# Attention, mixture of experts and MLP on one core: experts' results added to the tokens' rows in place, and the attention of four batches written out as one pipeline

## The reference

```python
# attention: B=4 batches, H=8 heads, S=576, D=64, stride 32
scores = q @ k.transpose(0, 1, 3, 2) / sqrt(D)
mask_local   = (rel >= 0) & (rel < 32)                  # heads 0..3
mask_strided = (rel >= 0) & (pos_k % 32 == pos_q % 32)  # heads 4..7
attn = softmax(where(mask, scores, -1e9)); x = attn @ v  # -> 2304 tokens x 512
# experts: E=8, D=512, F=1024
do_compute = (x @ w_skip) > 0
e_idx = argmax(x @ w_gate); gate_w = softmax(x @ w_gate)[e_idx]
x[do_compute] += gate_w * (relu(x @ w1[e_idx]) @ w2[e_idx])
# MLP, 512 -> 2048 -> 512
h = x @ w_in; out = maximum(0.01 * h, h) @ w_out
```

## Time and profile before

| | |
|---|---|
| median of 3 runs | 775.59 us (773.31 to 780.62) |
| the profiled execution | 770.11 us |
| its span, first to last instruction | 768.4 us |
| granted TensorE clock over the span | 0.970 |
| busy: PE, DVE, ACT, POOL | 94%, 36%, 32%, 24% |

### The profile page before, as it was taken

The page is one execution under the profiler, slowest core; times in us unless marked ns, Lnnn a source line. Parts: engine busy times, 40 slices in busy tenths (PEclk is TensorE's granted clock), DMA queues, the critical chain, the costliest instruction groups (busy, mean ns, idle before and its releaser), DMA issues.

```text
span 768.4 us, 12937 instructions
## 1 busy us (share of the span) xinstructions
PE 722.8 (94%) x4664; PEld 672.0 (87%) x4664; DVE 275.3 (36%) x589; ACT 242.0 (32%) x522; POOL 185.3 (24%) x190
## 2 busy tenths in 40 slices
PE   4999979894989999998999999999999999999997
PEld 3898879883989999997989999989998999899986
DVE  5757747657100000003332243233223323332222
ACT  3467656451111111123222322222222232223222
POOL 3120100102588777543000400130031004001000
PEclk9999989895899999999999999999999999999999
DMA  8473745772699999983000200030021003001001
GB/s 188 120 182 94 183 128 167 248 256 70 217 279 334 335 335 358 337 243 85 17 1 1 96 29 1 28 96 1 0 77 46 0 12 111 0 0 42 1 1 41
DMA packets 72441, 91.47 MB, mean 119 GB/s; under 512 B 26872, under 2 KB 47896, under 8 KB 72401
## 3 DMA queue, kind: packets, MB, share of 16 engines
q1 hardware_dynamic: 62289, 62.70, 27.7%
q0 software_dynamic: 9056, 28.23, 11.8%
q10 hardware_dynamic: 1056, 0.02, 0.1%
HBM read 73.91 MB, written 17.01 MB: 118 GB/s over the span
## 4 chain that ended last, share of the span: by engine, by line
PE 80%; SPq 10%; DMA 4%; issue 2%; DVE 2%; POOL 1%; ACT 1%; ACTq 0%; POOLq 0%; DVEq 0%
PE psum L1654 26%; PE psum L1673 26%; PE psum L1556 9%; PE psum L1572 8%; SPq L429 6%; SPq L424 2%; PE psum L1396 2%; DMA x_rows<-xo 2%; PE psum L1421 1%; PE psum L1512 1%; PE psum L1495 1%; SPq L414 1%; PE psum L1636 1%; DMA xg<-x_rows,idx 1%; PE psum L1582 1%
## 5 line engine op out<-in xcount | busy, mean ns | idle before, releaser
L1654 PE MATMUL psum<-x2h,wih 128*128 128x384 f32 x384 | 130.6, 340 | 1.9 <-DVE x2l L1316 1.9
L1334 DVE SCALAR_TENSOR_TENSOR g_act<-g_raw 128x384 f32<-128x384 f32 x96 | 53.6, 558 | 219.1 <-ACT g_raw L995 218.7
L1654 PE MATMUL psum<-x2h,wil 128*128 128x384 f32 x384 | 129.4, 337 | 0.0
L1654 PE MATMUL psum<-x2l,wih 128*128 128x384 f32 x384 | 128.9, 336 | 0.0
L995 ACT ACTIVATE g_raw<-psum 128x384 f32<-128x384 f32 x96 | 47.1, 491 | 235.0 <-PE psum L1654 235.0
L1673 PE MATMUL psum<-woh,g_l 128*128 128x512 f32 x288 | 114.0, 396 | 0.0
L1673 PE MATMUL psum<-wol,g_h 128*128 128x512 f32 x288 | 113.8, 395 | 0.0
L1673 PE MATMUL psum<-woh,g_h 128*128 128x512 f32 x288 | 112.2, 389 | 0.7 <-DVE g_l L1338 0.7
L1556 PE MATMUL psum<-xt,wring 128*128 128x160 f32 x512 | 82.6, 309 | 0.6 <-issue 0.6
L792 POOL DMA_INDIRECT out_dram<-o_sb,idxo x15 | 15.9, 1060 | 277.3 <-ACT o_sb L990 274.3
L1572 PE MATMUL psum<-hp,wring 128*128 128x160 f32 x512 | 78.5, 302 | 0.0
(11 more groups left out here) (197 smaller groups left out, 892.1 us busy)
## 6 DMA issues: line engine op xcount, KB each, us to landing
wring<-in_moe_w_dram SPq DMA_DIRECT2D x64, 512.0 KB, 9.8
q_st<-in_q_dram SPq DMA_DIRECT2D x8, 576.0 KB
k_st<-in_k_dram SPq DMA_DIRECT2D x8, 576.0 KB
x_sb<-x_rows SPq DMA_DIRECT2D x4, 1024.0 KB, 6.2
stage<-in_moe_w_in_dram POOLq DMA_DIRECT2D x4, 1024.0 KB, 10.1
stage<-in_moe_w_out_dram POOLq DMA_DIRECT2D x4, 1024.0 KB, 11.1
y_rows<-zrow POOLq DMA_DIRECT2D x7, 480.0 KB, 6.9
vs<-in_v_dram SPq DMA_DIRECT2D x20, 128.0 KB, 6.9
```

The source lines that it names most:

```text
L1334: dve.scalar_tensor_tensor(out=g_act[:, f % 2, :], in0=g_raw[:, f % 2, :], scalar=LEAK, in1=g_raw[:, f % 2, :], op0=ALU.mult, op1=ALU.max) ...
L1654: last = pe.matmul(bank[f % 2][:, 0:MT * P], wt[:, c, f * P:(f + 1) * P], xp[:, T.par, c, :], start=(c == 0 and n == 0), stop=(c == KD - 1 ...
```

## The change

**Attention.** The four batches are written out on all engines, with constant addresses and counts, and one rule for every batch: own chunks 8 to 15 two at a time ahead of groups 1 to 4 (`CH_AT`), the next batch's 0 to 7 ahead of groups 7 to 10 (`CH_NEXT`). The copies of a chunk (`chunk_copies`, both sides read in the order of the target) are the same text in both kernels. In batch 0, Q and K of the first four heads come as two pairs of heads, chunks 1, 3, 5, 7 are copied by DVE, V's first three loads stand ahead of the second half of Q and K, and that half is copied by POOL. Later DVE copies 9 and 13. POOL does all four copies into `q_in`/`k_in` of the later batches. The zeroing of half of `kt` moves from DVE to POOL. ACT waits for POOL's `zrow`, stores it as a row of zeros, and runs one exponential ahead of its first chunk; the split of the gate's weights moves behind group 1.

**Experts.** There is no `y_rows` and no zero fill. DVE multiplies a tile's result by the gate, adds it to the gathered rows `xg` (now two buffers) into `yr` (`x2_rows`), and POOL scatters `yr` into `x_rows` (`put_x`). The gates of all tiles come from three more groups of columns of the one-hot product at f = 8 of the first tile (before: 56 columns at f = 5, now 56 and 132). The next `x_turn` stands at f = 6, and the gather for it waits for `x2_rows` of the tile before. The sorted list holds only the token number, and DVE finishes it ahead of the one-hot forms. The MLP gathers one row instead of two; for the first 384 tokens it does so in POOL's last iteration.

```diff
@@ attention
-        CH_AT = {2: [12], 3: [13], 4: [14], 5: [15], 7: [0, 1], 8: [2, 3], 9: [4, 5], 10: [6, 7]}
-        ON_DVE = {9, 11}
+        CH_AT = {1: [8, 9], 2: [10, 11], 3: [12, 13], 4: [14, 15]}
+        CH_NEXT = {7: [0, 1], 8: [2, 3], 9: [4, 5], 10: [6, 7]}
+        def on_dve(b, n):
+            return n % 2 == 1 if b == 0 and n < 8 else n in (9, 13)
...
-            with sp.Fori(0, B - 2) as b:
-                batch(b, True, True)
-            batch(B - 2, False, True)
-            batch(B - 1, False, False)
...
+            pool.memset(kt[:, :, 2:4, :], 0.0).then_inc(s_kz, 1)
             step(pool.memset(zrow[:, :], 0.0))
...
+            act.wait_ge(s_cst, POOL_ZROW)
+            act.dma_start(x_flat[NONE:NONE + 1, :], zrow[:, :]).then_inc(s_zd, 16)
...
-                    if s_ in (6, 8) and not last:
-                        act.wait_ge(s_tq, len(CH) * b + len(CH))
-                        act.wait_ge(s_qs[1], 16 * b + 32)
-                        to, what = heads_in(q_in, q_st, 1)
...
-            act.wait_ge(s_wg, 32)
-            act.activation(wgs[:, :, 0:E + 1], wg[:, :, :], ACT.Copy).then_inc(s_wgh, 1)
+            act.wait_ge(s_vz, 1)
+            act.activation(warm[0:STRIDE, :], vs[0:STRIDE, 0, 0, 0:1], ACT.Exp)
             act.wait_ge(s_vz, 3)
...
@@ PE, attention
-            head(0)
-            with pe.Fori(0, B - 1) as b:
-                rest(b, False)
-                head(b)
-            rest(B - 1, True)
+            for b in range(B):
+                for g in range(NG):
+                    for n in CH_AT.get(g, []):
+                        chunk(b, n)
+                    for n in CH_NEXT.get(g, []):
+                        if b + 1 < B:
+                            chunk(b + 1, n)
+                    if g in (0, NL):
+                        copied(b, 15 if g else 7)
+                    scores(b, g)
+                    if NG * b + g >= 2:
+                        probs(*divmod(NG * b + g - 2, NG))
+                    if NG * b + g >= 3:
+                        values(*divmod(NG * b + g - 3, NG))
@@ POOL, experts
             for i in range(2 * NU):
-                pool.wait_ge(s_xt, 2 * (i + 1))
-                gather_x(i + 1)
+                if i == 0:
+                    pool.wait_ge(s_xt, 2)
+                    gather_x(1, 1)
+                else:
+                    if i == 1:
+                        pool.wait_ge(s_zd, 16)
+                    pool.wait_ge(s_x2r, 2 * i)
+                    if i + 1 < E:
+                        gather_x(i + 1, (i + 1) % 2)
+                    put_x(i - 1)
...
                 if i == 0:
-                    pool.wait_ge(s_tok_o, 1)
+                    pool.wait_ge(s_tok_o, 2)
+                if i == 2 * NU - 1:
+                    pool.wait_ge(s_srt, 16)
+                    indices(0)
+                    gather_rows(s_gm)
                 stage_split(i)
-                if i < ZPARTS:
-                    pool.dma_start(fill_rows(ZEARLY + ZPART * i, ZPART),
...
+                if i:
+                    put_done(i - 1)
@@ DVE, experts
+            def x2_rows(i, par, at_=2):
+                dve.wait_ge(s_yt, i * 2 + 2)
...
+                dve.wait_ge(s_yf, i + 1)
+                for hf in range(2):
...
+                    dve.scalar_tensor_tensor(out=yr[:, hf, :], in0=bank[at_ + hf][0:HALF, :],
+                                             scalar=gate2[:, hf:hf + 1], in1=x_, op0=ALU.mult,
+                                             op1=ALU.add).then_inc(s_x2r, 1)
@@ PE, experts
-                    if f == 3:
+                    if ahead and f == (3 if first else 6):
...
-                    if first and f == 5:
+                    if first and f == 8:
...
+                            last = pe.matmul(GATE_O.rearrange("p k h -> p (k h)"), row_o[:, t, :],
+                                             gate_o[:, t, :, :].rearrange("p k h -> p (k h)"),
                                              start=(t == 0), stop=(t == NT - 1))
```

More of the change, by code:

```diff
@@ L464, in x_load @@
+            qk_load(sp, 0, 1, k, k_st, s_ks[1])
+            for g in range(3, NL):
+                v_load(sp, 0, g)
+            qk_next(1, 0)
+            for g in range(NL, NG):
+                v_load(sp, 0, g)
+            qk_next(1, 1)
             def x_load(b):
@@ L769, in indices @@
-            def indices(m):
-                pool.tensor_copy(idx3[:, 0, :], column(m * MT, 0)).then_inc(s_i3, 1)
-                pool.tensor_copy(idx3[:, 1, :], column(m * MT, 1)).then_inc(s_i3, 1)
-                pool.wait_ge(s_i3, m * 2 + 2)
+            last_tile = pool.value_load(plan[0:1, 30:31], min_val=E - 1, max_val=TILES - 1)
+            with pool.If(tiles > E):
+                gather_x(E, 0)
+                with pool.Fori(0, NOV // 2) as i2:
+                    for u in range(2):
+                        i = i2 * 2 + (E + u)
+                        with pool.If(i < tiles):
+                            pool.wait_ge(s_x2r, i * 2)
+                            carry()
+                            gather_x(i + 1, 1 - u)
+                            put_x(i - 1)
+                            put_done(i - 1)
+                        with pool.Else():
+                            pass
+                pool.wait_ge(s_x2r, tiles * 2)
@@ L783, in scatter_out @@
+                gather_rows(s_gr)
+                for j in range(MT):
+                    pool.wait_ge(s_gr[j], 16)
+                pool.sem_inc(s_rd, 1)
+            with pool.Else():
+                pool.sem_inc(s_rd, 1)
+                pool.wait_ge(s_x2r, 2 * E)
+                put_x(E - 1)
+                put_done(E - 1)
             def scatter_out(m):
-                pool.tensor_copy(idxo[:, :], column(m * MT, 0)).then_inc(s_io, 1)
+                pool.tensor_copy(idxo[:, :], column(m * MT)).then_inc(s_io, 1)
@@ L942, in tile @@
                                    ).then_inc(s_hp, 1)
-                    if f == 4:
+                    if ahead and f == (4 if first else 6):
                         x_copy(T.i0 + (T.d + 1), 1 - par)
-                    if f == 1 and not first:
-                        y_rows(T.i0 + (T.d - 1))
                 act.wait_ge(s_l2, T.n(FC, FC))
@@ L1341, in mstep @@
                         outputs(T)
-                    if not last and f == 5:
-                        x2_rows(T.i0 + (T.d + 1))
                     if not last and f in (8, 10, 12):
@@ L1432, in head @@
-            def head(b):
-                before = not isinstance(b, int)
-                new = b + 1 if before else b
-                for n in (8, 9):
-                    chunk(new, n)
-                if before:
-                    probs(b, NG - 2)
-                    values(b, NG - 3)
-                for n in (10, 11):
-                    chunk(new, n)
-                if before:
-                    probs(b, NG - 1)
-                copied(new, 7)
-                scores(new, 0)
-                if before:
-                    values(b, NG - 2)
-                scores(new, 1)
-                if before:
-                    values(b, NG - 1)
@@ L1453, in rest @@
-            def rest(b, last):
-                for s_ in range(2, NG):
-                    if s_ == NL:
-                        copied(b, 15)
-                    for n in CH_AT.get(s_, []):
-                        if n >= 8:
-                            chunk(b, n)
-                        elif not last:
-                            chunk(b + 1, n)
-                    scores(b, s_)
-                    probs(b, s_ - 2)
-                    if s_ >= 3:
-                        values(b, s_ - 3)
@@ L1616, in _ @@
                     tile(Tile(i2 * 2, u + 1))
-            tile(Tile(0, E - 1))
+            tile(Tile(0, E - 1), False)
             with pe.If(tiles > E):
+                for hf in range(2):
+                    pe.wait_ge(s_xf[hf], E)
+                pe.wait_ge(s_x2r, 2 * (E - 1))
+                x_turn(E, 0)
                 with pe.Fori(0, (NOV + 3) // 4) as i4:
@@ L1629, in _ @@
                         pass
+                for hf in range(2):
+                    pe.wait_ge(s_xf[hf], tiles + 1)
             with pe.Else():
@@ L1663, in mshare @@
                     pe.wait_ge(s_stl, 2 * NU)
-                    for hf in range(2):
-                        pe.wait_ge(s_xf[hf], tiles * 2 + 1)
+                    pe.wait_ge(s_x2r, tiles * 2)
                 if f == 0 and not T.first:
```

669 lines of the change are left out of this document (322 added, 347 removed).

## The result

The changed kernel takes 802.9 us (median of 4 runs, 794.8 to 806.6) against 775.4 for the kernel before on the same chip: 1.033 times as long, interval 1.023 to 1.043. Forecast were 759.6 and a range of 750 to 771. The profiled execution is the shortest of the four, 794.84 us for a span of 792.9; before, the span was 768.4.

What follows compares the result with a forecast made beforehand. PE was taken to bound MLP, experts and batch 3, leaving attention, the second tile and the way into the MLP. 15.5 - 1.1 + 2.1 - 0.5 = 16.0 us less: 775.6 to 759.6, range 750 to 771.

Steps and rivals of the forecast that it cites:

- For every later tile ... Cost 0.: Experts, tiles after the second: gathers land in time, POOL and PE fit with 1 us to spare; cost 0, end -3.
- slower: the ring in the experts: Rival, experts: each gather's second half lands 2 us late for `x_turn`, 4.3 us a tile; 785 us, chance 0.05.
- Sum for attention: ... 15.5. Nothing hides this: Attention: start and four batches together gain 15.5 us, all reaching the routing, which begins when the last `xo` is there.
- SP falls behind no further: Attention, batch 2: SP needs 26 us a batch and PE 28.0, so 38.5 becomes 28.0; gain 10.5 us.
- stores still late: Rival, attention: SP's queue still governs batches 1 and 2, stores landing near 9.4 us; 768.0 us, chance 0.13.
- Opening: Start of attention: DVE shares the chunk copies with ACT, first group at 17.5 instead of 19.0; gain 1.5 us.
- slow opening: Rival, start of attention: POOL's zeroing takes 7.0 us, all chunks begin 4.5 us later; 764.1 us, chance 0.09.
- Batch 0: Attention, first batch: PE's 2.90 us wait for ACT goes, 33.0 becomes 27.4 us; gain 5.6.
- Batch 1: Attention, second batch: a 2.3 us wait for a store and a slow clock, 31.3 us against 30.2; loss 1.1.
- First tile: Experts, first tile: 132 more columns of the one-hot product on PE, all on the path; loss 1.1 us.
- Second tile: Experts, second tile: later gather but later `x_turn`, wait about 1.7 us, 2.2 lost instead of 4.3; gain 2.1.
- Into the last stage: From experts into MLP: ACT's copies go, DVE's additions come, PE waits for POOL's signal; loss 0.5 us.

Runs made afterwards that it cites:

- rows16: The changed kernel with rows of `sorted_rows` widened from 4 to 16 bytes: 776.9 us, 1.006 times the kernel before.
- before_v_pool: The kernel before, with V of each batch's last three strided groups (12 of 20 loads) issued by POOL instead of SP: 754.4 us, ratio 0.978.

## Why the prediction was wrong

The forecast of 16.0 us less became 24.7 more in the profiled execution. Two steps failed: in both I put a cost at nothing.

**"For every later tile ... Cost 0."** The transfers were counted by megabytes ("the zero fills, 0.48 MB a tile ... are gone, which speaks for early landings"), and the diff's narrower `sorted_rows` appeared only as three columns at the cost of their issue. It saves no work worth naming and holds up the engines, for 9 us on end in the stretch shown. `rows16` puts it at 2.7% of the time, some 21 us. The remaining 3.3 us of the experts are the stop behind the turn, which no row of before could show; moving the turn ends it. The rival "slower: the ring in the experts" had the place, the experts, but the wrong mechanism: X's turn waited once, 0.91 us, and the tiles waited for weights. Its 785 was nearer by chance.

**"Sum for attention: ... 15.5. Nothing hides this", and for batch 2 "SP falls behind no further".** SP did. I had its 26 us a batch against PE's 28.0, too close to be trusted, and it needs 32.7 and 29.2. In the first of these a store of three local tiles took 3.35 us to issue and the six local loads of V 5.3, where I counted half a microsecond each, and SP stood still for 1.0; in the second the six loads took 4.6 and two loads of the experts' weights, which I had left out, 1.4. That the routing begins "when the last `xo` is there" was right. What I did not follow is that this last `xo` itself waits for a store, issued at 140.70 behind all of SP's V loads and landed 8.8 us later. PE ended attention at 145.0 instead of 147.6 and waited 5.77 us. The rival "stores still late" had this mechanism, for batches 1 and 2: stores landed after 6.9 us in the median and 13.4 at worst, against the 6.4 and 9.4 of the earlier trace rows. But it let 7.1 us through, and next to nothing came through before SP was relieved. `before_v_pool` shows the size of what SP holds: 15.6 us.

Step by step for the rest:
- Opening, forecast +1.5 (first group at 17.5): it came at 20.28, 1.2 later than before. POOL zeroed `kt` in 2.12 us with DVE idle beside it, near the 2.1 I had as one end, so the rival "slow opening" with its 7.0 is out. ACT did begin at 11.6 (forecast 11.2). What I missed is that the second pair of heads comes in behind it on DVE, whose copy took 2.23 us instead of 0.68. The timelines of POOL and DVE after:

```profile
7.05 2.12 POOL L621 MEMSET kt<- 128x2432 f32 x1
...
14.04 1.89 POOL L657 COPY q_in<-q_st 72x2048 f32<-72x2048 f32 x1 [2.85 <-DMA q_st<-in_q_dram]
```

```profile
14.25 2.23 DVE L1082 COPY q_in<-q_st 72x1024 f32<-72x1024 f32 x1
16.40 0.68 DVE L1082 COPY k_in<-k_st 72x1024 f32<-72x1024 f32 x1
```

- DVE's copy of 2.23 us began under POOL's and ended at 16.48, 0.55 behind its end. This agrees with the prediction's rule (the Trainium skill, "SBUF — State Buffer", section "SBUF: two separate sides"): the later one is blocked for the whole instruction. I applied it to POOL's zeroing and not to the copies that POOL now does in the same stretch.
- Batch 0, forecast 27.4: 30.1. The wait of 2.9 for ACT went as forecast; the groups are not shorter. Batch 1, forecast 31.3: 29.8, without a long wait. Batch 2, forecast 28.0: 35.4, with a wait of 3.02 us for a store at 84.9 and a clock of 0.90 behind it, as the earlier trace rows had it before. It went as the rival said. Batch 3, forecast 27.7 (26.7 and 1.0): 29.4.
- First tile, forecast -1.1 for the one-hot product of the gates: it stands from 210.97 to about 212.7, 0.9 more than the 0.84 of the earlier trace rows. Right.
- Second tile, "x_turn" at 227.2 and its gather at 228.9: 232.5, and 233.8 for the second half. POOL's first split ended at 221.2, as forecast (221); but `x2_rows`, taken at 1.8 us, took 5.5, since its small copy of the gates lay under that split:

```profile
217.19 4.05 DVE L1286 COPY gate<-gate_s 80x2 f32 x1 [2.12 <-PE psum L1561]
221.27 1.41 DVE L1293 SCALAR_TENSOR_TENSOR yr<-psum,gate,xg 80x512 f32<-80x512 f32 x2
```

- Into the last stage, forecast -0.5: from the last turn of Y to the first matmul 4.75 us (374.10 to 378.85) against 4.27 (349.94 to 354.21). Right.

## What to carry to other kernels

A narrower record is not a cheaper one. Rows of 4 bytes side by side cost up to 4.9% here; rows of 16 bytes side by side, or of 4 bytes 64 apart, cost under 1%. Price each changed layout apart from the bytes it moves. Before a gain is added up engine by engine, follow each queue that issues transfers to its last instruction, and each wait to the transfer behind it; a queue that is almost never idle can hide every gain before it, as SP's did here. And try first whether the queue can be relieved: twelve loads a batch given to another engine brought 15.6 us, as much as a new order of the whole pipeline was meant to bring.

## What the runs showed of the hardware

- A scatter of 4-byte rows packed 4 bytes apart holds up the loads beside and behind it, those of other queues too: the DMA share is 1.00 at 57 GB/s, and loads of 1 MB take longer to land. The issues of the experts' stage, first before, then after (last number: median us to landing):

```profile
stage<-in_moe_w_in_dram POOLq DMA_DIRECT2D x3, 1024.0 KB, 10.6
```

```profile
stage<-in_moe_w_in_dram POOLq DMA_DIRECT2D x3, 1024.0 KB, 17.7
```

- The Trainium skill, "DMA: Bandwidth & Descriptors", section "Issuing engines are not separate DMA queues", holds that issuing from several engines saves only the issue time, "which is usually small relative to the DMA itself". Here SP issues 26 loads of V a batch, the small ones at about 0.8 us each, and giving twelve of them to POOL, with the same bytes moved, was worth 15.6 us over four batches in the kernel before. The issue time is not shown to be all of it: the stores left in SP's queue landed after 4.5 us in the median instead of 6.4.
- DVE's copy of 80 x 2 elements took 4.05 us under POOL's subtraction of 4.50 us, and 0.17 in the seven other tiles of the same run.
